# Normalising a tile's hidden values ahead of, and not behind, splitting the next attention pair

## The chip, the cores and the metric

The kernel runs on one core of a Trainium2 chip. Its engines work in parallel, each through its own list of instructions in order: TensorE (PE; PEld is its weight load), VectorE (DVE), ScalarE (ACT), GpSimd (POOL), and SyncE (SP), which issues the DMAs. They meet through semaphores. The metric is the device time of one execution in microseconds, median of several.

## The reference

Windowed attention, then two gated layers, all in fp32:

```python
# attention: 2 batches, 8 heads, 768 positions, head size 64
scores = scale * q @ k.T + bias            # kept: 8 global keys and 96 local ones
a = softmax(scores); attn_out = a @ v
# layer 1: x is [1536, 512], w_in [512, 1024], w_out [1024, 512]
h = x @ w_in
solu = h * softmax(h)
ln = (solu - mean(solu)) / sqrt(var(solu) + 1e-6) * g_ln
y = ln @ w_out
# layer 2: w_gate, w_val [512, 1536], w_down [1536, 512]
yn = y / sqrt(mean(y * y) + 1e-6) * rms_g
out = (silu(yn @ w_gate) * (yn @ w_val)) @ w_down
```

## The kernel before

The 1536 rows are 12 tiles of 128 rows. A first stage does attention and layer 1, tile by tile; a second does layer 2 in 6 blocks of two tiles. Each product of fp32 values is made of three products of parts: a value is rounded to a shorter form (`hi`, on ACT), the rest is `lo = value - hi` (on DVE, "split"), and PE adds hi\*hi, hi\*lo and lo\*hi.

In the first stage, `one_tile(t)` on each engine walks over four steps p = 0 to 3, one for each pair of heads. It is software-pipelined by hand: the attention belongs to tile a = t + 1, the hidden layer to tile t, and the layer norm and the second product of layer 1 to tile t - 1. The order of the calls in `one_tile` is the order of each engine's queue; nothing reorders it. Tiles 2 to 7 run in a loop, the others are written out. In tiles 1 and 8 to 11 DVE also splits weights (`split_block`).

What touches the change, on its engines:

- DVE `take_logits(n + 1)` (L974) takes the scores of a pair out of PSUM, adds the bias and finds the row maximum.
- DVE `split_qk(n + 2)` (L951 and L952) makes `k_lo`, and the rest of the queries in `qk_hi`, of the pair after the next. It waits for ACT's rounding (`qk_rounded`). PE's `score_pair` (L1202, L1203) of that pair waits for it (`qk_split`), and opens the next step p on PE.
- DVE `take_variance(t - 1)` at p = 0 ends in a first guess of one over the square root (L1040). POOL's `newton` (L577, L580, L583, three rounds, then L587) refines it on one column and gives the factor `col[:, 7:8]`.
- DVE `apply_norm(t - 1)` (L1045), at p = 1, waits for that factor and normalises `gated`, 128 x 1024, in place.
- PE `turn_ln(t - 1, 0)` (L1271), at p = 2 right behind `score_pair`, transposes `gated`; ACT and DVE (`split_ln`, L1050) then form `ln_hi` and `ln_lo` for the product with `w_out`.
- PE at p = 1 and 2 also makes the hidden products (`ffn_in`, L399 to L401); at p = 3 it transposes `recip_wide` (L1243). `ffn_out` and `mix_pair` (L1230) fill the rest.

Of the kernel before, what the change touches and what calls it, by code (L numbers as in the profile page):

```python
# [41 lines left out]
def fused_kernel(nc, qk_pairs, v_windows, n_global, n_local,  # L42
# [47 lines left out]
    with whole:  # L90
# [205 lines left out]
        def known(t):  # L296
            return isinstance(t, int)

        def settle(engine, t):


            if not known(t):
                engine.sem_inc(settled, 1)

        def is_tile(t):
            return not known(t) or 0 <= t < tiles
# [508 lines left out]
        def _(dve):  # L815
# [129 lines left out]
            def split_qk(n, p):  # L945

                if not is_pair(n):
                    return
                dve.wait_ge(qk_rounded, n + 1)
                hi = qk_hi[:, p % 2].bitcast(F32)  # L950
                nc.vector.tensor_tensor(k_lo[:, p % 2], qk_raw[:, p, 0:KEYS], hi[:, 0:KEYS], ALU.subtract)  # L951
                nc.vector.tensor_tensor(qk_hi[d:, p % 2, KEYS:], qk_raw[d:, p, KEYS:], hi[d:, KEYS:],  # L952
                                        ALU.subtract).then_inc(qk_split, 1)

            def take_logits(n, even, p):

                if not is_pair(n):
                    return
                dve.wait_ge(scores_ready, n + 1)
                if even == 0 and p == 0 and (not known(n) or n > 0):  # L960
                    dve.wait_ge(bias_set, n // (2 * pairs))
                if known(n) and n < pairs:
                    dve.wait_ge(bias_first, 2 * (p + 1))
                if known(n) and n == pairs:
                    dve.wait_ge(bias_others, heads)
                for h in range(2):
                    if not known(n) or n >= 2:
                        dve.wait_ge(probs_ready, 2 * (n - 2) + h + 1)
                    settle(dve, n)
                    head = 2 * p + h  # L970
                    b = bias_even[:, head] if even == 0 else bias[:, 1, head]
                    if known(n) and n < pairs:
                        b = bias[:, 0, head]
                    nc.vector.tensor_tensor_reduce(logits[:, 2 * (p % 2) + h], scores[h][:, 0:WIN], b,  # L974
                                                   -S_SCALE, 3.0e38, ALU.add, ALU.min,
                                                   neg_max[:, even, head:head + 1]).then_inc(logits_ready, 1)

            def invert_sums(a, even):
                dve.wait_ge(probs_ready, heads * (a + 1))
                nc.vector.tensor_scalar(denom[:], exp_sum[:, even], 1e-9, None, ALU.add).then_inc(denom_steps, 1)  # L980
                dve.wait_ge(denom_steps, 3 * a + 1)
                nc.vector.reciprocal(recip[:], denom[:]).then_inc(denom_steps, 1)
                dve.wait_ge(denom_steps, 3 * a + 2)
                if not known(a) or a >= 1:
                    dve.wait_ge(recip_turned, a)
                nc.vector.tensor_copy(recip_wide[:], recip[:].unsqueeze(2).to_broadcast([P, heads, d])
                                      ).then_inc(denom_steps, 1)

            def normalise_x(a):
                dve.wait_ge(recip_copied, a + 1)  # L990
                dve.wait_ge(mixed_ready, pairs * (a + 1))
                nc.vector.tensor_tensor(x[:], mixed[:].rearrange("p (c n) -> p c n", c=pairs), x[:],
                                        ALU.mult).then_inc(x_ready, 1)
# [6 lines left out]
            def max_hidden(t, n):  # L1000
                dve.wait_ge(hidden_ready, N1 * t + n + 1)
                nc.vector.tensor_reduce(h_max[:, n:n + 1], hidden[:, n], AX_X, ALU.max).then_inc(max_steps, 1)
                if n == N1 - 1:
                    dve.wait_ge(max_steps, 3 * t + 2)
                    nc.vector.tensor_scalar(h_neg[:], h_max[:, 0:1], h_max[:, 1:2], -1.0, ALU.max, ALU.mult
                                            ).then_inc(max_steps, 1)
# [18 lines left out]
            def take_variance(t):  # L1025
                at = LN_STEPS * t
                dve.wait_ge(ln_steps, at + 4)
                settle(dve, t)
                nc.vector.bn_aggr(moments[:], stats[:]).then_inc(ln_steps, 1)
                dve.wait_ge(ln_steps, at + 5)  # L1030

                nc.vector.tensor_scalar(col[:, 2:3], moments[:, 1:2], col[:, 1:2], col[:, 1:2],
                                        ALU.mult, ALU.mult).then_inc(ln_steps, 1)
                dve.wait_ge(ln_steps, at + 6)
                nc.vector.tensor_scalar(col[:, 3:4], col[:, 2:3], 1e-6, None, ALU.add).then_inc(ln_steps, 1)
                dve.wait_ge(ln_steps, at + 7)
                nc.vector.tensor_scalar(seed_bits[:, 0:1], col[:, 3:4].bitcast(I32), 1, None,
                                        ALU.logical_shift_right).then_inc(ln_steps, 1)
                dve.wait_ge(ln_steps, at + 8)
                nc.vector.tensor_scalar(seed_bits[:, 1:2], seed_bits[:, 0:1], -1.0, RSQRT_SEED,  # L1040
                                        ALU.mult, ALU.add).then_inc(seed_ready, 1)

            def apply_norm(t):
                dve.wait_ge(rstd_ready, t + 1)
                nc.vector.tensor_scalar(gated[:], gated[:], moments[:, 0:1], col[:, 7:8],  # L1045
                                        ALU.subtract, ALU.mult).then_inc(ln_ready, 1)

            def split_ln(t, n):
                dve.wait_ge(ln_rounded, N1 * t + n + 1)
                nc.vector.tensor_tensor(ln_lo[:, n * KJ:(n + 1) * KJ], turned_x[:].rearrange("p (k n) -> p k n", k=KJ),  # L1050
                                        ln_hi[:, n * KJ:(n + 1) * KJ].bitcast(F32),
                                        ALU.subtract).then_inc(ln_split, 1)
# [42 lines left out]
            def one_tile(t, even):  # L1095
                a = t + AHEAD
                for p in range(pairs):
                    n = pairs * a + p
                    if p == 0 and is_tile(t):
                        normalise_x(t)  # L1100
                    if p == 3 and is_tile(t):
                        max_hidden(t, 1)
                    take_logits(n + 1, 1 - even if p < pairs - 1 else even, (p + 1) % pairs)
                    if p == 3 and is_tile(a):
                        invert_sums(a, 1 - even)
                    if p == 0 and is_tile(t - 1):
                        take_variance(t - 1)
                    if p == 2 and is_tile(t - 1):
                        split_ln(t - 1, 0)
                    if p == 2 and is_tile(t):  # L1110
                        max_hidden(t, 0)
                    split_qk(n + 2, (p + 2) % pairs)
                    if p == 1 and is_tile(t - 1):
                        apply_norm(t - 1)
                    if p == 0 and is_tile(t):
                        split_x(t, even)
                    if known(t) and t == tiles - 1 and p == 2:
                        normalise_y(0, 0)
                    if p == 2 and is_tile(t - 1):
                        split_ln(t - 1, 1)  # L1120
                    if known(t) and t == tiles - 1 and p == 3:
                        split_y(0, 0, 0)
                    if p == 3 and is_tile(t):
                        gate_hidden(t)
                        measure_hidden(t)
                    if known(t) and t == -AHEAD and p == 0:
                        start_distance(1)
                        finish_distance(1)
                    if known(t) and t == tiles - 4 and p == 1:
                        scale_of_y(0)  # L1130
                    if known(t) and t == tiles - 1 and p == 3:
                        split_y(0, 1, 0)
                        take_variance(t)
                    for c, half in split_1.get((t, p), ()) if known(t) else ():
                        split_block(dve, c, half)
# [340 lines left out]
```

## Time and profile before

| | us |
|---|---|
| median of three runs (597.48 to 598.37) | 598.06 |
| the profiled execution's own time | 598.06 |
| its span, first to last instruction | 596.2 |
| PE busy | 555.7 |
| DVE busy | 308.3 |
| ACT busy | 264.8 |
| POOL busy | 84.4 |

Busy times are of one profiled execution. The first stage lasts until about 275 us in it, the second from there to the end. In a timeline, a bracket behind a row gives how long the engine was idle before it and whose end released it. A busy time of PE counts overlapping matmuls once.

### The profile page before, as it was taken

The page shows a single profiled execution, that of the slowest core. Times are in us where ns is not written, and L with a number is a line of the kernel's source. Part 1 is how long each engine was busy: PE and PEld are TensorE (multiplying, and loading weights), DVE is VectorE, ACT ScalarE, POOL GpSimd, SP SyncE. Part 2 cuts the span into 40 slices and gives each one's busy share as a digit, 9 for nine tenths or more (in the row PEclk, how much of TensorE's full clock was granted, in tenths as well). Part 3 has the DMA queues.
Part 4 walks back from the last instruction along what each step waited for, and adds up shares of the span by engine and source line. Part 5 has one row for each costly group of instructions (what it writes and reads, how often), then busy time and mean ns, then how long its engine had stood idle before and what let it go on. Part 6 is the DMA issues. An engine that isn't in the chain of part 4 may idle for free.

```text
span 596.2 us, 10724 instructions
## 1 busy us (share of the span) xinstructions
PE 555.7 (93%) x3696; PEld 479.1 (80%) x3696; DVE 308.3 (52%) x798; ACT 264.8 (44%) x609; POOL 84.4 (14%) x215
## 2 busy tenths in 40 slices
PE   2368899999999999999999999999999999999997
PEld 1246677777777777768899999999999999999996
DVE  5578788778877898767455213222222222231211
ACT  2557656766776777656454212221222222222112
POOL 1240220322122205323010010001001000100000
PEclk9969799999999999999999999999999999999999
DMA  7767564433443333232532100010020000001000
GB/s 171 190 169 169 155 176 123 124 108 91 123 124 110 92 123 100 94 119 81 184 108 89 48 25 1 1 70 1 1 70 0 0 0 35 0 0 37 2 1 35
DMA packets 22965, 46.95 MB, mean 79 GB/s; under 512 B 4128, under 2 KB 4128, under 8 KB 22928
## 3 DMA queue, kind: packets, MB, share of 16 engines
q1 hardware_dynamic: 22928, 46.48, 26.8%
q8 instruction: 20, 0.33, 0.2%
q14 instruction: 17, 0.14, 0.1%
HBM read 40.18 MB, written 6.29 MB: 78 GB/s over the span
## 4 chain that ended last, share of the span: by engine, by line
PE 79%; DVE 9%; POOL 3%; issue 3%; DMA 3%; ACT 2%; SPq 1%; DVEq 0%; ACTq 0%
PE hidden L399 9%; PE hidden L400 8%; PE hidden L401 8%; PE mixed L1230 4%; PE turned L399 3%; PE scores_a L399 3%; PE mixed L399 3%; PE turned L400 3%; PE scores_b L399 3%; PE mixed L400 3%; PE turned L401 3%; PE scores_a L400 3%; PE scores_b L400 3%; PE scores_b L401 3%; PE scores_a L401 3%
## 5 line engine op out<-in xcount | busy, mean ns | idle before, releaser
L718 ACT ACTIVATE act_hi<-act_sb 128x256 fp32r<-128x256 f32 x72 | 30.1, 418 | 108.3 <-DVE act_sb L1087 108.3
L1087 DVE TENSOR_TENSOR act_sb<-mixed,silu 128x256 f32<-128x256 f32 x36 | 15.3, 425 | 93.9 <-PE mixed L401 93.5
L1087 DVE TENSOR_TENSOR act_sb<-turned,silu 128x256 f32<-128x256 f32 x36 | 15.3, 424 | 89.1 <-PE turned L401 86.5
L399 PE MATMUL hidden<-down_hi,act_hi 128*128 128x512 f32 x144 | 57.1, 397 | 0.1
L400 PE MATMUL hidden<-down_lo,act_hi 128*128 128x512 f32 x144 | 56.9, 395 | 0.0
L401 PE MATMUL hidden<-down_hi,act_lo 128*128 128x512 f32 x144 | 56.7, 394 | 0.0
L662 ACT ACTIVATE probs_t<-turned 116x512 f32<-116x512 f32 x48 | 28.6, 595 | 49.7 <-PE turned L1215 49.6
L1092 DVE TENSOR_TENSOR act_lo<-act_sb,act_hi 128x256 fp32r<-128x256 f32 x72 | 30.6, 425 | 34.9 <-ACT act_hi L718 34.9
L652 ACT ACTIVATE probs<-logits,neg_max 128x232 f32<-128x232 f32 x96 | 45.6, 480 | 3.2 <-DVE neg_max L974 3.2
L1230 PE MATMUL mixed<-probs_t,v_in 116*64 116x128 f32 x384 | 33.9, 301 | 11.9 <-ACT probs_t L662 10.4
L1230 PEld LDWEIGHTS mixed<-probs_t,v_in 116*64 116x64 f32 x384 | 21.6, 145 | 28.7 <-issue 15.1
L642 ACT ACTIVATE qk_hi<-qk_raw 128x720 fp32r<-128x720 f32 x48 | 38.1, 794 | 14.2 <-DMA qk_raw<-qk_pairs 14.2
L399 PE MATMUL hidden<-in_hi,xt_hi 128*128 128x512 f32 x96 | 42.7, 445 | 0.0
L399 PE MATMUL turned<-yt_hi,val_hi 128*128 128x256 f32 x144 | 40.9, 284 | 0.0
L399 PE MATMUL mixed<-yt_hi,val_hi 128*128 128x256 f32 x144 | 40.9, 284 | 0.0
L399 PE MATMUL scores_a<-yt_hi,gate_hi 128*128 128x256 f32 x144 | 40.5, 281 | 0.0
L400 PE MATMUL mixed<-yt_lo,val_hi 128*128 128x256 f32 x144 | 40.4, 281 | 0.0
L400 PE MATMUL turned<-yt_lo,val_hi 128*128 128x256 f32 x144 | 40.4, 281 | 0.0
L400 PE MATMUL scores_b<-yt_lo,gate_hi 128*128 128x256 f32 x144 | 40.4, 281 | 0.0
L400 PE MATMUL scores_a<-yt_lo,gate_hi 128*128 128x256 f32 x144 | 40.4, 281 | 0.0
L401 PE MATMUL turned<-yt_hi,val_lo 128*128 128x256 f32 x144 | 40.4, 281 | 0.0
L399 PE MATMUL scores_b<-yt_hi,gate_hi 128*128 128x256 f32 x144 | 40.4, 281 | 0.0
(142 smaller groups left out, 1556.1 us busy)
## 6 DMA issues: line engine op xcount, KB each, us to landing
qk_raw<-qk_pairs SPq DMA_DIRECT2D x96, 180.0 KB, 3.3
v_in<-v_windows SPq DMA_DIRECT2D x12, 464.0 KB
staging<-w_gate SPq DMA_DIRECT2D x3, 1024.0 KB, 6.9
staging<-w_val SPq DMA_DIRECT2D x3, 1024.0 KB, 6.9
y_spill<-y_out SPq DMA_DIRECT2D x12, 256.0 KB, 7.6
staging<-w_down SPq DMA_DIRECT2D x3, 1024.0 KB, 5.5
y_in<-y_spill SPq DMA_DIRECT2D x6, 512.0 KB, 4.1
out<-o_sb SPq DMA_DIRECT2D x12, 256.0 KB, 2.1
```

The costliest lines, as they stand in the source:

```text
L399: pe.matmul(acc, hi, other_hi, start=first, stop=False)
L400: pe.matmul(acc, hi, other_lo, start=False, stop=False)
L401: return pe.matmul(acc, lo, other_hi, start=False, stop=last)
L642: nc.scalar.activation(qk_hi[:, p % 2], qk_raw[:, p], ACT.Copy).then_inc(qk_rounded, 1)
L652: nc.scalar.activation(probs[:, p % 2, h], logits[:, 2 * (p % 2) + h], ACT.Exp, bias=neg_max[:, even, head:head + 1], scale=-1.0, accum_ou ...
L662: nc.scalar.activation(probs_t[:, p % 2], turned[0:HALF, :], ACT.Copy).then_inc(probs_t_ready, 1)
L718: nc.scalar.activation(act_hi[:, slot], act_sb[:, slot], ACT.Copy).then_inc(act_rounded, 1)
L1087: nc.vector.tensor_tensor(act_sb[:, slot], val_ps[slot][:, 0:WIDE], silu[:, slot], ALU.mult).then_inc(act_ready, 1)
L1092: nc.vector.tensor_tensor(act_lo[:, slot], act_sb[:, slot], act_hi[:, slot].bitcast(F32), ALU.subtract).then_inc(act_split, 1)
L1230: ins = pe.matmul(mixed[h * d:(h + 1) * d, p * P:(p + 1) * P], v_in[:, even, half, head * d:(head + 1) * d], probs_t[:, p % 2, h, half], s ...
```

## The change

In DVE's `one_tile` the call of `apply_norm(t - 1)` at p = 1 moves from behind `split_qk` to ahead of it. Both still come after `take_logits`, each keeps its own waits, and no other engine's list is touched.

```diff
                     if p == 0 and is_tile(t - 1):
                         take_variance(t - 1)
+                    if p == 1 and is_tile(t - 1):
+                        apply_norm(t - 1)
                     if p == 2 and is_tile(t - 1):
                         split_ln(t - 1, 0)
                     if p == 2 and is_tile(t):
                         max_hidden(t, 0)
                     split_qk(n + 2, (p + 2) % pairs)
-                    if p == 1 and is_tile(t - 1):
-                        apply_norm(t - 1)
```

DVE's list in the loop (tiles 2 to 7), at p = 1, the half with the even tiles' bias; the rows with - are where they stood before, those with + where they stand now:

```order
 L974 ISA logits,neg_max<-scores_b,bias_even 128x232 [waits probs_ready]
 L974 ISA neg_max 128x1
+L1045 TENSOR_SCALAR gated<-gated,moments,col 128x1024 [waits rstd_ready]
 L949 REGISTER_ALU
 L951 TENSOR_TENSOR k_lo<-qk_raw,qk_hi 128x464 [waits qk_rounded]
 L952 TENSOR_TENSOR qk_hi<-qk_raw,qk_hi 64x256
-L1045 TENSOR_SCALAR gated<-gated,moments,col 128x1024 [waits rstd_ready]
 L968 ISA [waits scores_ready]
 L974 ISA logits,neg_max<-scores_a,bias_even 128x232 [waits probs_ready]
```

The instruction that waits for POOL (`rstd_ready`) now stands ahead of the two that split the pair.

DVE's list in tile 9, at p = 1, where weights are split behind it:

```order
 L974 ISA logits,neg_max<-scores_b,bias_even 128x232 [waits probs_ready]
 L974 ISA neg_max 128x1
-L951 TENSOR_TENSOR k_lo<-qk_raw,qk_hi 128x464 [waits qk_rounded]
-L952 TENSOR_TENSOR qk_hi<-qk_raw,qk_hi 64x256
 L1045 TENSOR_SCALAR gated<-gated,moments,col 128x1024 [waits rstd_ready]
+L951 TENSOR_TENSOR k_lo<-qk_raw,qk_hi 128x464 [waits qk_rounded]
+L952 TENSOR_TENSOR qk_hi<-qk_raw,qk_hi 64x256
 L380 SCALAR_TENSOR_TENSOR val_lo<-staging,rms_col,val_hi 128x512 [waits w_rounded]
 L380 SCALAR_TENSOR_TENSOR val_lo<-staging,rms_col,val_hi 128x512
```

The same swap; the weights' split keeps its place behind both. PE's list is the same before and after. A `score_pair` in it, in the loop, as it stands in both:

```order
L1198 ISA [waits qk_split]
L1202 MATMUL scores_a<-qk_hi 128x232 [waits logits_ready]
L1203 MATMUL scores_a<-k_lo,qk_hi 128x232
L1198 REGISTER_ALU
L1202 MATMUL scores_b<-qk_hi 128x232 [waits logits_ready]
L1203 MATMUL scores_b<-k_lo,qk_hi 128x232
```

Nothing moved here; this is the place on PE that waits for what DVE's L952 signals.

## Rows read from the trace of the kernel before

**Rows 1.** The page: busy us (share of the span) xinstructions; then the chain.
```profile
PE 555.7 (93%) x3696; PEld 479.1 (80%) x3696; DVE 308.3 (52%) x798; ACT 264.8 (44%) x609; POOL 84.4 (14%) x215
...
PE 79%; DVE 9%; POOL 3%; issue 3%; DMA 3%; ACT 2%; SPq 1%; DVEq 0%; ACTq 0%
```

**Rows 2.** Windows: start:end, length, busy us of each engine, PEclk, DMA share, GB/s.
```profile
100.00:150.00 50.00, 49.60 (x319) 38.04 (x318) 40.27 (x114) 33.31 (x84) 14.42 (x31) 1.00 0.37 108
```

**Rows 3.** Waits around L1045: its own, then those for its output (us, times).
```profile
  POOL col L587: 17.5, 12
who waited for it (us, times):
  PEld turned_x L1271: 3.4, 3
  PE turned_x L1271: 2.4, 3
```

**Rows 4.** Timeline of DVE, tile 5: start us, us, operation, [idle before <-releaser].
```profile
146.42 0.64 DVE L951 TENSOR_TENSOR k_lo<-qk_raw,qk_hi 128x464 fp32r<-128x464 f32 x1
147.07 0.42 DVE L952 TENSOR_TENSOR qk_hi<-qk_raw,qk_hi 64x256 fp32r<-64x256 f32 x1
148.78 0.81 DVE L1045 TENSOR_SCALAR gated<-gated,moments,col 128x1024 f32<-128x1024 f32 x1 [1.28 <-POOL col L587]
```

**Rows 5.** Timeline of POOL, tile 5, and the same steps beside idle DVE, tile 11.
```profile
146.54 0.67 POOL L583 TENSOR_SCALAR col<-col 128x1 f32<-128x1 f32 x1
147.31 0.40 POOL L577 TENSOR_SCALAR col<-col 128x1 f32<-128x1 f32 x1
147.80 0.19 POOL L580 TENSOR_SCALAR col<-col 128x1 f32<-128x1 f32 x1
...
263.15 0.28 POOL L583 TENSOR_SCALAR col<-col 128x1 f32<-128x1 f32 x1
263.54 0.33 POOL L577 TENSOR_SCALAR col<-col 128x1 f32<-128x1 f32 x1
263.96 0.19 POOL L580 TENSOR_SCALAR col<-col 128x1 f32<-128x1 f32 x1
```

**Rows 6.** Timelines of DVE and PE: start-up, then PE in tile 5.
```profile
62.80 0.42 DVE L952 TENSOR_TENSOR qk_hi<-qk_raw,qk_hi 64x256 fp32r<-64x256 f32 x1
...
63.28 0.56 PE L1202 MATMUL scores_a<-qk_hi 128*128 128x232 f32 x1 [1.40 <-DVE qk_hi L952]
...
149.45 0.38 PE L1202 MATMUL scores_a<-qk_hi 128*128 128x232 f32 x1
...
150.00 0.60 PE L1271 MATMUL turned_x<-ident,gated 128*128 128x128 f32 x4
```

**Rows 7.** Timelines of DVE and PE, tile 1, at the swapped place.
```profile
67.65 0.81 DVE L1045 TENSOR_SCALAR gated<-gated,moments,col 128x1024 f32<-128x1024 f32 x1 [1.12 <-POOL col L587]
...
69.64 0.38 PE L1202 MATMUL scores_a<-qk_hi 128*128 128x232 f32 x1
```

**Rows 8.** Timelines of DVE and PE, tiles 8 to 10.
```profile
207.93 0.81 DVE L1045 TENSOR_SCALAR gated<-gated,moments,col 128x1024 f32<-128x1024 f32 x1 [0.84 <-POOL col L587]
...
211.85 0.66 PE L1271 MATMUL turned_x<-ident,gated 128*128 128x128 f32 x4 [0.41 <-DVE ln_lo L1050]
...
228.90 0.81 DVE L1045 TENSOR_SCALAR gated<-gated,moments,col 128x1024 f32<-128x1024 f32 x1 [1.66 <-POOL col L587]
229.63 1.41 DVE L380 SCALAR_TENSOR_TENSOR val_lo<-staging,rms_col,val_hi 128x512 fp32r<-128x512 f32 x2
230.95 0.39 DVE L974 CUSTOM_DVE_ANT_0 logits<-scores_a,bias_even 128x232 f32<-128x232 f32 x1
...
229.77 0.66 PE L1271 MATMUL turned_x<-ident,gated 128*128 128x128 f32 x4 [0.70 <-DVE gated L1045]
...
248.56 0.81 DVE L1045 TENSOR_SCALAR gated<-gated,moments,col 128x1024 f32<-128x1024 f32 x1 [1.11 <-POOL col L587]
```

## The prediction

> **What bounds the kernel now.** I first read the page's busy times and its chain of waits [rows 1]: TensorE (PE) is busy 93% of the span and holds 79% of the chain that ended last, VectorE (DVE) 9%, GpSimd (POOL) 3%. Then the windows, to see whether that holds where the change is made: between 100 and 150 us PE is busy 49.60 of 50 us, at a granted clock of 1.00, DVE 40.27 of 50 [rows 2]. So in the steady tiles PE has almost no holes, and any hole that the change opens in PE's stream is added to the time, while a microsecond saved on DVE alone is worth nothing. The third view is who waits around the moved instruction [rows 3]: before the 12 runs of `apply_norm` DVE stands idle for 17.5 us in all, each time until POOL's last Newton operation, L587. PE and its weight load wait for what `apply_norm` writes only at three places each, 2.4 and 3.4 us. The reader should see that `apply_norm` starts when POOL lets it, not when DVE gets to it.
>
> The timeline of tile 5 shows how that looks [rows 4]. DVE starts the key split (`k_lo`) at 146.42, its second half `qk_hi` at 147.07, and is through at 147.07 + 0.42 = 147.49. Then it idles 1.28 us, and `apply_norm` runs from 148.78 for 0.81. PE takes the product of the pair just split at 149.45 and the transposes of `gated` at 150.00 [rows 6]. So the split is done 149.45 - 147.49 = 1.96 us before PE wants it: this is the slack that the change spends.
>
> **The change, part by part.** Nothing is added or removed. The two split instructions go behind the wait for POOL and behind `apply_norm`, in tiles 1 to 10, ten times (in tile 11 no pair is left to split). Queued behind the wait on DVE are then the split, through it PE's next `score_pair`, and behind that on PE the transposes, the products with `w_in` and everything else, since PE works in order. Where the code prepares weights (tiles 1 and 8 to 10), the splits of those are behind it on DVE too.
>
> *When does `apply_norm` start now?* Were POOL not to change, at the same 148.78, since it was waiting already. But POOL's chain has two stretched places while the split runs beside it [rows 5]: from the L583 at 146.54 to the next start at 147.31 is 0.77 us, and on to 147.80 is 0.49. The same two steps where DVE is idle (263.15 to 263.54 to 263.96) take 0.39 and 0.42. After the change DVE is idle during them, so I take 0.38 + 0.07 = 0.45 us off. The bounds are zero (DVE's split was not what stretched them) and 1.07 (the whole length of the split, 147.49 - 146.42). I take 0.45, since it is a difference of rows of the very same two steps. So `apply_norm` starts at 148.78 - 0.45 = 148.33.
>
> I use starts of consecutive POOL instructions, not their durations. The Trainium skill (Perfetto Trace Analysis, GPSIMD Engine Instruction) advises exactly that, calling the profiled span of a GpSimd instruction unreliable; here the durations in the same rows would give 0.39 + 0.07 = 0.46, so nothing hangs on it.
>
> *When does PE get the pair?* The instruction after `apply_norm` starts 0.73 us after it (228.90 to 229.63 [rows 8]). The split takes 1.07 as above. From its end to PE's start is 0.06: in the start-up stretch, where PE did wait for it, `qk_hi` ended at 62.80 + 0.42 = 63.22 and PE began at 63.28 [rows 6]. So PE starts 0.73 + 1.07 + 0.06 = 1.86 us after `apply_norm` starts: 148.33 + 1.86 = 150.19, against 149.45. That is +0.74 us.
>
> *Does it come back later in the tile?* PE's loss at this place moves PE's later products, DVE's logits that wait for them, the hidden products and with these the sums, the seed and POOL's next Newton chain by the same amount; I see no clock in the loop that runs on by itself (its DMA loads are a tile ahead). The waits of PE for `recip_wide` move with PE's own scores. So nothing is given back in tiles 2 to 7, six tiles alike: 6 x 0.74 = 4.4 us.
>
> *Tile 1.* PE takes its pair at 69.64 while `apply_norm` started at 67.65 [rows 7]. Even with no relief on POOL, 67.65 + 1.86 = 69.51 is before 69.64: cost zero. The cover is 0.13 us, and with POOL's relief some 0.6.
>
> *Tiles 8 to 10.* Here DVE also rounds off weights for the next stage, and is nearly as late as PE. `apply_norm` is at 207.93, 228.90 and 248.56; in tile 9 two weight splits follow at 229.63 and the logits at 230.95 without a pause [rows 8]. What stands behind the swapped group moves by the split's 1.07 less POOL's 0.45, that is 0.62 us. PE meets its pair some 0.9 to 1.1 us later, but it had holes there already, 0.41 us at 211.85 (on `ln_lo`) and 0.70 at 229.77 (on `gated`), which swallow the difference. What passes through is DVE's 0.62: 3 x 0.62 = 1.9 us. The bounds are zero (holes and DVE slack take it all) and 1.07 each.
>
> *Sum.* 0 + 4.4 + 1.9 = 6.3 us on a profiled span of 596.2. The profiled execution took 598.06, which is also the median of the runs shown, with 1.86 outside the span. So 598.06 + 6.3 = 604.4 us, or +1.1%.
>
> **The rivals.**
>
> *POOL is not relieved.* If the stretched steps have another cause, `apply_norm` stays at its times, and tiles 2 to 7 cost 148.78 + 1.86 - 149.45 = 1.19 each, tiles 8 to 10 1.07 each: 7.1 + 3.2 = 10.3, so 608.4 us. For it: POOL's other long steps don't all sit beside a split. Against it: the same steps in the stretch with idle DVE are short. Chance 0.10.
>
> *The late tiles absorb theirs.* Then only 4.4 us remain: 602.5. For it: DVE and PE both have holes in tiles 8 to 10. Chance 0.08.
>
> *POOL is relieved by the whole split.* Tiles 2 to 7 would cost 1.19 - 1.07 = 0.12 each, the late ones nothing: 0.7 us, so 598.8 and no measurable change. Against it: the two steps are stretched by 0.45 in all, and a relief can't give back more than was taken. Chance 0.03. The Trainium skill (SBUF — State Buffer, Who interferes with whom) has a DVE instruction with two SBUF inputs, as both splits are, contend with a GpSimd instruction that reads SBUF, the loser of a shared port blocking fully rather than sharing; were POOL held for all of the split, this rival would follow, but the rows show it held for less than half.
>
> *Faster.* If POOL's result were there by the time DVE has its logits, 146.42, `apply_norm` would not wait, PE's transposes would find `gated` earlier, and DVE would lose its holes of the late tiles (0.84, 1.66 and 1.11 us before the three rows of `apply_norm` [rows 8]). That is 3.6 us at most, since PE hides DVE's holes elsewhere: 594.5. It decides at a relief of 148.78 - 146.42 = 2.36 us on POOL, and against the 0.45 seen there is no sign of it; already for a tie in the steady tiles 1.19 would be needed. Chance 0.02. That the order isn't changed at all is out: DVE's program shows the swap at all its places, with PE's untouched.
>
> *More than that.* Something behind PE's hole could add to it (a weight load not hidden, ScalarE's queue of exponentials getting late). The nearest row is the transposes after a wait, 0.66 us at 229.77 against 0.60 at 150.00: below 0.1 us a tile, which carries it to 605.3. The chance for a time beyond 608.4 I put at 0.04.
>
> **How the numbers follow.** The forecast, 604.4, has 0.73; its own range is 603.4 to 605.8. The range that holds the time 8 times in 10 takes in the late tiles absorbed at its lower end (602.5, a little below for rounding: 602.2) and reaches toward the unrelieved POOL at its upper end (608.4): 602.2 to 608.4. A measurement of this kernel can tell about 0.2%, 1.2 us, from no change. Only the fully relieved POOL lies within it, 0.03; only its early result is faster, 0.02; the rest, 0.95, is slower.
>
> **What would show it.** Right: in tiles 2 to 7 the wait of `k_lo` disappears behind `apply_norm`, DVE's idle before `apply_norm` grows from 1.28 to about 148.33 - 146.42 = 1.9 us, PE shows a hole of 0.7 us before `score_pair` of the last pair, released by `qk_hi` L952, in about nine tiles, and POOL's steps L583 and L577 take 0.39 and 0.42. Wrong: no such hole (the split is still in time), POOL's steps as long as before (then 608), or a later wait in the tile, such as the one for `recip_wide`, shrinking by what PE lost.

## The result, and the profile after

| | before | changed |
|---|---|---|
| median, us | 597.77 (597.32 to 598.37) | 604.23 (604.19 to 604.97) |
| profiled execution, span, us | 596.2 | 603.7 |
| PE busy, us | 555.7 | 557.3 |
| DVE busy, us | 308.3 | 308.5 |
| POOL busy, us | 84.4 | 79.1 |

The changed kernel takes 1.011 of the time before, 95% interval 1.0093 to 1.0128. The forecast was 604.4, and slower. The profiled execution of the changed kernel took 605.45, 1.2 us over its median; the section after the experiments says what such differences are.

The page of the changed kernel, busy times and chain, to be held against [rows 1]:

```profile
PE 557.3 (92%) x3696; PEld 480.5 (80%) x3696; DVE 308.5 (51%) x798; ACT 264.8 (44%) x609; POOL 79.1 (13%) x215
...
PE 65%; DVE 15%; POOL 8%; issue 6%; DMA 3%; ACT 1%; SPq 1%; DVEq 0%; ACTq 0%; POOLq 0%
```

No engine has more than 1.6 us of work added (PE), but the chain no longer stays on PE: its share falls from 79% to 65%, and DVE and POOL rise from 9% and 3% to 15% and 8%. That is what it looks like when two side engines become links of the loop. Where PE had hardly any holes [rows 2] it has them now; the same window (length, busy us of PE, PEld, DVE, ACT, POOL, clock, DMA share, GB/s):

```profile
100.00:150.00 50.00, 48.00 (x303) 36.94 (x304) 40.21 (x114) 32.13 (x80) 11.76 (x27) 1.00 0.37 104
```

PE is busy 48.00 us in place of 49.60 at the same clock. The holes are in one place of each tile. Tile 5 of the changed kernel in the timelines of DVE, POOL and PE, answering to [rows 4 to 6]:

```profile
151.73 0.81 DVE L1045 TENSOR_SCALAR gated<-gated,moments,col 128x1024 f32<-128x1024 f32 x1 [1.81 <-POOL col L587]
152.46 0.64 DVE L951 TENSOR_TENSOR k_lo<-qk_raw,qk_hi 128x464 fp32r<-128x464 f32 x1
153.11 0.42 DVE L952 TENSOR_TENSOR qk_hi<-qk_raw,qk_hi 64x256 fp32r<-64x256 f32 x1
...
149.94 0.28 POOL L583 TENSOR_SCALAR col<-col 128x1 f32<-128x1 f32 x1
150.33 0.33 POOL L577 TENSOR_SCALAR col<-col 128x1 f32<-128x1 f32 x1
150.75 0.19 POOL L580 TENSOR_SCALAR col<-col 128x1 f32<-128x1 f32 x1
...
152.26 0.66 PE L1230 MATMUL mixed<-probs_t,v_in 116*64 116x128 f32 x8
153.66 0.37 PE L1202 MATMUL scores_a<-qk_hi 128*128 128x232 f32 x1 [0.74 <-DVE qk_hi L952]
```

Read from the bottom: PE idles 0.74 us until `qk_hi`; that split ends at 153.11 + 0.42 = 153.53, and it stood behind `apply_norm`, which had waited 1.81 us for POOL. The split itself needed nothing of POOL. POOL's two steps take 0.39 and 0.42 us from start to start, against 0.77 and 0.49 in [rows 5].

What PE loses here is a little more than the bracket says. In the kernel before, the scores of this pair (149.45 in [rows 6]) stood behind

```profile
148.86 0.66 PE L1230 MATMUL mixed<-probs_t,v_in 116*64 116x128 f32 x8
```

that is 0.59 us from start to start. Now it is 153.66 - 152.26 = 1.40, 0.81 more. The bracket of 0.74 counts from the end of the `mixed` products in the record, 0.66 after their start.

Two stretches of PE's timeline measure the cost without the start-up: A from the scores of step 1 of tile 2 to those of step 1 of tile 8, which holds the six swaps of the loop, and B from there to the first transposes of the last tile's `gated`, which holds the three late ones and all that follows in the first stage. The three ends in the kernel before, then in the changed one:

```profile
85.14 0.37 PE L1202 MATMUL scores_a<-qk_hi 128*128 128x232 f32 x1
203.87 0.38 PE L1202 MATMUL scores_a<-qk_hi 128*128 128x232 f32 x1
284.20 0.66 PE L1271 MATMUL turned_x<-ident,gated 128*128 128x128 f32 x4 [0.67 <-DVE gated L1045]
```
```profile
86.09 0.37 PE L1202 MATMUL scores_a<-qk_hi 128*128 128x232 f32 x1
209.74 0.38 PE L1202 MATMUL scores_a<-qk_hi 128*128 128x232 f32 x1
291.62 0.66 PE L1271 MATMUL turned_x<-ident,gated 128*128 128x128 f32 x4 [0.66 <-DVE gated L1045]
```

A went from 118.73 to 123.65, that is +4.92 or 0.82 a tile, and B from 80.33 to 81.88, +1.55. Together 6.5 us, as the medians have it (604.23 - 597.77 = 6.46); the second measurement of the same kernel (e12 below) has 6.2 in A and B and 7.4 by the medians. What follows B, to the end, is 312.0 us before and 312.1 after: nothing comes back. The same two stretches, read in the same way, in all kernels:

| kernel | A, us | B, us | median - median before, us |
|---|---|---|---|
| before | 118.73 | 80.33 | |
| changed, first | 123.65 | 81.88 | +6.5 |
| e12_changed_again | 123.66 | 81.65 | +7.4 |
| e1_loop | 123.62 | 80.33 | +6.4 |
| e2_late | 118.76 | 83.47 | +4.8 |
| e3_first | 118.75 | 80.40 | +0.8 |
| e10_tiles_8_10 | 118.73 | 81.42 | +0.5 |
| e11_tile_9 | 118.72 | 80.90 | +1.1 |
| e4_two_inputs | 125.53 | 83.49 | +10.2 |
| e5_one_input | 123.55 | 81.89 | +7.1 |
| e6_after_two_rounds | 118.71 | 76.96 | -2.4 |
| e7_before_two_rounds | 118.74 | 76.29 | -2.7 |
| e8_turn_first | 121.63 | 81.70 | +3.8 |
| e9_weights_first | 118.79 | 82.01 | +4.0 |

### The profile page after: what moved, and what is told of

It reads as the page before. It is cut to its first block, busy times and chain, and to the rows that moved or that the text cites. A ratio compares the mean times of both kernels' runs of the same rounds, so it can differ in the third digit from the quotient of the medians.

```text
span 603.7 us, 10724 instructions
## 1 busy us (share of the span) xinstructions
PE 557.3 (92%) x3696; PEld 480.5 (80%) x3696; DVE 308.5 (51%) x798; ACT 264.8 (44%) x609; POOL 79.1 (13%) x215
## 4 chain that ended last, share of the span: by engine, by line
PE 65%; DVE 15%; POOL 8%; issue 6%; DMA 3%; ACT 1%; SPq 1%; DVEq 0%; ACTq 0%; POOLq 0%
PE hidden L399 8%; PE hidden L400 7%; PE hidden L401 7%; POOL col L577 3%; PE turned L399 3%; PE mixed L399 3%; PE turned L401 3%; PE turned L400 3%; PE mixed L400 3%; PE scores_b L399 3%; PE scores_a L399 3%; PE scores_b L400 3%; PE scores_a L400 3%; PE scores_a L401 3%; PE scores_b L401 3%
## 5 line engine op out<-in xcount | busy, mean ns | idle before, releaser
L1230 PE MATMUL mixed<-probs_t,v_in 116*64 116x128 f32 x384 | 34.0, 301 | 11.7 <-ACT probs_t L662 10.2
L401 PE MATMUL scores_b<-yt_hi,gate_lo 128*128 128x256 f32 x144 | 40.4, 280 | 0.0
```

The lines of the kernel that those rows point to most:

```text
L401: return pe.matmul(acc, lo, other_hi, start=False, stop=last)
L1230: ins = pe.matmul(mixed[h * d:(h + 1) * d, p * P:(p + 1) * P], v_in[:, even, half, head * d:(head + 1) * d], probs_t[:, p % 2, h, half], s ...
```

## The experiments

### Which tiles pay: the swap in parts

The swap was made under a condition, here for the loop; the others have `known(t) and t >= 8`, `t == 1`, `t in (8, 10)` and `t == 9`:

```diff
+                    if p == 1 and is_tile(t - 1) and (not known(t)):
+                        apply_norm(t - 1)
 ...
                     split_qk(n + 2, (p + 2) % pairs)
+                    if p == 1 and is_tile(t - 1) and not (not known(t)):
+                        apply_norm(t - 1)
```

> The swap in tiles 2 to 7 alone (the loop). My theory: each tile costs PE what it lost in the changed kernel's trace, a hole of 0.74 us before the last pair's scores and a distance of 0.82 us from tile to tile, so 6 x 0.82 = 4.9 us over the kernel before, about +0.8%, and nothing comes back later. Rival, recovery: tiles 8 to 11 have holes of their own (0.41, 0.70 and 0.98 us on PE) and swallow up to 2.1 us of it: +2.8 to 3 us.

Measured: 604.02 against 597.64 us, ratio 1.01 (1.0084 to 1.0116). In the trace A is 4.89 us longer and B is that of before. Six tiles cost 0.82 each and none of it is recovered. The median says 6.4, 1.5 more; in the traced execution these 1.5 lie ahead of the swapped tiles, in the start-up (below).

> The swap in tile 1 alone. My theory: no cost, the split is still done before TensorE wants it; 0.0 us, at most 0.2 either way. Rival: the 0.29 us by which tile 1 was longer in the changed kernel's trace belong to the swap: +0.3 us. (In that trace another 0.67 us had gone by before tile 1, in the start-up, where nothing was changed; I hold that for the difference of two executions.)

Measured: 598.41 against 597.64, ratio 1.0009 (0.9999 to 1.0019), with A and B within 0.1 us of before. Its `apply_norm` started at 67.29 and the split ended at 69.09, and PE took its scores at 69.96 without a wait. Tile 1 costs nothing: the cover held.

> The swap in tiles 8 to 10 alone. My theory: VectorE's split of 1.07 us comes behind the wait, less what POOL is relieved, 0.5 to 0.6 us a tile in the changed kernel's trace, so +1.6 us, about +0.27%. Rival, absorbed: the holes that TensorE had there take it, and the time is that of before within 0.3 us. Rival, TensorE's holes count in full (0.73, 1.71 and 0.75 us before the scores in the changed kernel's trace): +3.2 us.

Measured: 602.44 against 597.64, ratio 1.0075 (1.0062 to 1.0089). Here the theory missed: B is 3.14 us longer, and not 1.55 as in the changed kernel, whose code for these tiles is the same. The whole difference is in tile 9. The rows of this run, PE in tile 9:

```profile
231.01 0.37 PE L1204 MATMUL scores_a<-qk_hi 128*128 128x232 f32 x1 [1.71 <-DVE qk_hi L952]
...
231.60 1.06 PE L1273 MATMUL turned_x<-ident,gated 128*128 128x128 f32 x4
232.31 0.78 PE L399 MATMUL hidden<-in_hi,xt_hi 128*128 128x512 f32 x1
232.88 0.63 PE L400 MATMUL hidden<-in_lo,xt_hi 128*128 128x512 f32 x1
```

and its windows, where the granted clock is the third number from the end:

```profile
231.00:232.00 1.00, 0.98 (x6) 0.99 (x7) 1.00 (x2) 0.00 (x0) 0.84 (x3) 0.75 0.00 0
232.00:233.00 1.00, 1.00 (x6) 0.90 (x5) 1.00 (x5) 0.31 (x1) 0.82 (x3) 0.50 0.70 181
233.00:234.00 1.00, 1.00 (x4) 0.81 (x3) 0.72 (x4) 0.98 (x2) 0.67 (x5) 0.50 1.00 288
```

PE's hole of 0.70 us on `gated` in tile 9 [rows 8] is gone, one of 1.71 us stands before the scores, and behind it the granted clock is 0.50 (1.2 in place of 2.4 GHz): the same products take 0.63 us in place of 0.39. In the changed kernel's first profile the hole was 1.71 us as well, and the clock stayed at 1.00:

```profile
237.50:238.50 1.00, 1.00 (x7) 0.83 (x6) 1.00 (x4) 0.75 (x2) 0.82 (x3) 1.00 0.61 190
```

Three more runs take this apart.

> The swap in tiles 8 and 10 alone, to take apart the run with the swap in tiles 8 to 10, which cost 4.8 us by the medians where 1.6 was expected, and in whose trace TensorE ran tile 9's hidden products after a hole of 1.71 us at a granted clock of 0.50. Theory now: the extra is that stretch at half clock, and it belongs to tile 9's hole. So here there is no such stretch: 0.57 + 0.44 = 1.0 us over the kernel before, a granted clock of 1.00 all through 200 to 300 us. Rival: each of the three late swaps costs some 1.5 us: +3.0 us.

> The swap in tile 9 alone. Theory: a hole of about 1.7 us on TensorE before the last pair's scores, which costs 0.54 us as such, and, where the granted clock falls to 0.50 behind it, 1.6 us more: +2.1 us in those executions. Rival, no clock in it: +0.5 us. Rival, a third of the 4.8 us: +1.6 us without a stretch at 0.50.

> The changed kernel again, with the swap at all ten places. In its first profiled execution tile 9's hole was 1.71 us too, but the granted clock stayed at 1.00 behind it. Theory: six tiles at 0.82 and three late ones at 0.52 us, 6.5 us over the kernel before (604.1 to 604.6), and whether the clock falls in tile 9 differs from execution to execution; where it does, 1.6 us more. Rival: the parts add up (6.4 us for the loop and 4.8 us for the late tiles by the medians), 11 us, and the first measurement was a lucky one.

Measured: 598.85, 599.53 and 605.82 against 598.39 us; ratios 1.0009 (1.0 to 1.0017), 1.001 (1.0001 to 1.002) and 1.0113 (1.0096 to 1.013). In the traces B is 1.09 us longer with tiles 8 and 10, 0.57 with tile 9 alone, and 1.32 with all, none with a stretch at 0.50. The rival by which the parts add up to 11 us has fallen. Tile 9 alone, with the hole and without the fall:

```profile
231.18 0.37 PE L1204 MATMUL scores_a<-qk_hi 128*128 128x232 f32 x1 [1.68 <-DVE qk_hi L952]
...
232.40 0.39 PE L400 MATMUL hidden<-in_lo,xt_hi 128*128 128x512 f32 x1
```

So a late swap costs about 0.5 us, and the 1.6 us on top are TensorE's clock, which fell behind that hole in two traces (e2_late, e4_two_inputs; holes of 1.71 and 1.69 us) and not in four others (1.71, 1.70, 1.68 and 1.42). What decides it is open, and no two traces of one kernel show both. The mean granted clock of each execution, which is on record without a trace too, hints that one kernel can do both: two executions of e4_two_inputs stand at 0.992 and took 608.89 (the traced one) and 609.34 us, two at 0.994 and took 607.24 and 607.00. The slow stretch of its trace, 239.4 to 242.9 us, lowers such a mean by 0.003.

### What stretches POOL

```diff
+                    if p == 1 and not known(t):
+                        dve.wait_ge(qk_rounded, n + 3)
+                        hi = qk_hi[:, (p + 2) % 2].bitcast(F32)
+                        raw = qk_raw[:, (p + 2) % pairs]
+                        nc.vector.tensor_tensor(spare[:, 0:KEYS], raw[:, 0:KEYS], hi[:, 0:KEYS], ALU.subtract)
+                        nc.vector.tensor_tensor(spare[d:, KEYS:QK], raw[d:, KEYS:], hi[d:, KEYS:], ALU.subtract)
                     if p == 1 and is_tile(t - 1):
                         apply_norm(t - 1)
```

> The changed kernel, plus in tiles 2 to 7 a copy of the pair's split into unused memory (two VectorE subtractions, 128x464 and 64x256, each with two inputs in SBUF) at the place where the split stood before, ahead of the wait for POOL. VectorE was idle there for 1.8 us and the copy takes 1.07, so VectorE has the time. My theory: POOL's steps L583 and L577 are stretched again by 0.45 us as in the kernel before, the normalisation is that much later, and each of six tiles costs 0.45 more: 2.7 us over the changed kernel, some 606.9 us, +1.5% over the kernel before. Rival: POOL's stretched steps had another cause, and the time stays at that of the changed kernel, +1.1%.

and, in its place, one instruction with one input:

```diff
+                        nc.vector.tensor_reduce(spare[:, 0:1], qk_raw[:, (p + 2) % pairs], AX_X, ALU.max)
```

> The changed kernel, plus in tiles 2 to 7 a maximum over 128x720 (one input in SBUF, about 0.95 us) at the place of the extra subtractions of the run with two inputs. My theory: it is the second SBUF input of the split that stretches POOL, so this one leaves POOL's steps at 0.39 and 0.42 us from start to start, and the time stays at the changed kernel's, +1.1%. Rival: any VectorE work beside POOL stretches it, +1.5% as with two inputs.

Measured: 608.07 and 604.98 against 597.89 us, ratios 1.0163 (1.0136 to 1.0189) and 1.0109 (1.0086 to 1.0132). DVE and POOL in tile 5, first with two inputs, then with one:

```profile
150.62 0.64 DVE L1112 TENSOR_TENSOR spare<-qk_raw,qk_hi 128x464 f32<-128x464 f32 x1
151.27 0.42 DVE L1113 TENSOR_TENSOR spare<-qk_raw,qk_hi 64x256 f32<-64x256 f32 x1
...
150.76 0.65 POOL L583 TENSOR_SCALAR col<-col 128x1 f32<-128x1 f32 x1
151.51 0.40 POOL L577 TENSOR_SCALAR col<-col 128x1 f32<-128x1 f32 x1
152.00 0.19 POOL L580 TENSOR_SCALAR col<-col 128x1 f32<-128x1 f32 x1
```
```profile
149.43 0.90 DVE L1110 TENSOR_REDUCE spare<-qk_raw 128x1 f32<-128x720 f32 x1
...
149.57 0.28 POOL L583 TENSOR_SCALAR col<-col 128x1 f32<-128x1 f32 x1
149.96 0.33 POOL L577 TENSOR_SCALAR col<-col 128x1 f32<-128x1 f32 x1
150.38 0.19 POOL L580 TENSOR_SCALAR col<-col 128x1 f32<-128x1 f32 x1
```

Beside two inputs POOL's steps are 0.75 and 0.49 us from start to start, beside one 0.39 and 0.42, as if DVE were idle. That settles the term of 0.45. The two instructions also differ in what they write, 464 values in a partition against one. Writing by itself didn't stretch POOL at another place: in the kernel before, `take_logits` (L974, 145.78 to 146.50), with one input in PSUM, one in SBUF and 232 values written to SBUF, ran beside POOL's L577 and L580, and they took 0.42 and 0.29 us from start to start, as in tile 11 beside an idle DVE. The cost was less than expected: A grew by 125.53 - 123.65 = 1.9 us, not 2.7. PE's hole grew from 0.74 to 1.17 on average, the full 0.43, but in the even tiles a later wait, that of PE's L1243 for `recip_wide`, shrank: from 0.58, 0.31 and 0.30 us in tiles 2, 4 and 6 to 0.21, 0.20 and 0.20. The rest of this run's excess is its half-clock stretch in tile 9 (B is 1.6 longer than the changed kernel's).

### Is it the wait for POOL?

```diff
-                for s in range(NEWTON):
+                for s in range(LN_NEWTON):
```

with LN_NEWTON = 2 in place of NEWTON = 3, so that the normalisation's root has one round less of refinement; first in the changed order, then in the order of before.

> The changed kernel with two Newton rounds on POOL in place of three for the layer norm (one round left out, so the factor is less precise), which brings POOL's result 1.09 us earlier. My theory: the hole of 0.74 us on TensorE is the wait for POOL handed on through the split, so it is gone in all tiles where it was, and the time is that of the kernel before with two rounds within 0.5 us, near 597, not above 598.5. Rival: the cost comes from VectorE's order alone (the split simply later by the 0.81 us of the normalisation): then at least two thirds of the 6.5 us stay, 602 or more.

> The kernel before with two Newton rounds in place of three (one left out). My theory: in tiles 1 to 8 and 10 nobody on the chain waits for POOL, and only TensorE's three holes on the normalised values go (0.70 in tile 9, 0.98 in tile 11, 0.67 after it), so 595.5 to 597.5. Rival: POOL's chain bounds nothing, 597.8 as before. With the run of the changed kernel and two rounds it shows what the swap costs when POOL is early.

Measured: 595.49 and 595.24 against 597.89, ratios 0.9964 (0.9948 to 0.9979) and 0.9952 (0.9934 to 0.997). With POOL's result 1.09 us earlier the swap costs 0.0 us in A (118.71 against 118.74) and 0.7 in B, where tile 9 keeps a hole of 0.60. PE in tile 5 of the changed order with two rounds has no bracket:

```profile
146.25 0.81 DVE L1046 TENSOR_SCALAR gated<-gated,moments,col 128x1024 f32<-128x1024 f32 x1 [0.72 <-POOL col L588]
...
148.46 0.37 PE L1203 MATMUL scores_a<-qk_hi 128*128 128x232 f32 x1
```

DVE still waits 0.72 us there, and nobody minds: the split is done at 148.04 and PE comes at 148.46. The order is harmless where the thing waited for comes early enough. They gain 3.4 and 4.0 us in B over the kernel before, more than the 2.35 that the three holes at `gated` gave reason to expect. In the order of before, the 0.41 on `ln_lo` in tile 8 goes too, and each hole was worth more than its bracket: tile 8 is 0.65 us shorter, tile 9 1.09 for its 0.70, and the rest of B 2.30 for 0.98 + 0.67.

### Giving PE something to do in the hole

```diff
+                    if p == 2 and is_tile(t - 1):
+                        turn_ln(t - 1, 0)
                     score_pair(n + 1, (p + 1) % pairs)
                     if p == 0 and is_tile(t - 2):
                         ffn_out(t - 2, range(4, 6))
-                    if p == 2 and is_tile(t - 1):
-                        turn_ln(t - 1, 0)
```

> The changed kernel, with TensorE's order changed to fit it: at the third step of a tile the four transposes of the normalised values (0.44 us) go ahead of the scores of the last pair. They need the normalisation, which the change puts ahead of the split. My theory: they run in the hole, which shrinks from 0.74 to about 0.3 us, so six tiles gain 0.44 each and tiles 8 to 10 up to as much: 2.6 to 3.9 us less than the changed kernel, 600.3 to 601.6, still above the kernel before. Rival: the scores don't get later but what follows does (VectorE's logits, the rounding on ScalarE of the transposed values), and the gain is under 1 us.

Measured: 602.11 against 598.31, ratio 1.0061 (1.0043 to 1.008). A is 2.0 us shorter than in the changed kernel, B 0.2: the right mechanism, but 2.2 us and not 2.6 to 3.9. PE in tile 5:

```profile
150.72 0.66 PE L1230 MATMUL mixed<-probs_t,v_in 116*64 116x128 f32 x8
151.31 0.66 PE L1271 MATMUL turned_x<-ident,gated 128*128 128x128 f32 x4
152.12 0.37 PE L1202 MATMUL scores_a<-qk_hi 128*128 128x232 f32 x1 [0.16 <-DVE qk_hi L952]
```

The hole is 0.16 in place of 0.74, but the scores come no earlier: 152.12 - 150.72 = 1.40 us behind the start of `mixed`, as in the changed kernel. What is saved is the time that the transposes took behind them. In the changed kernel that was 0.35 us from their start to the next product (154.21 to 154.56), not 0.44; A is 0.34 a tile shorter. The late tiles gain almost nothing, since DVE's order decides there.

### Other work ahead of the wait

```diff
+                    for c, half in split_1.get((t, p), ()) if known(t) and p == 1 else ():
+                        split_block(dve, c, half)
                     if p == 1 and is_tile(t - 1):
                         apply_norm(t - 1)
 ...
-                    for c, half in split_1.get((t, p), ()) if known(t) else ():
+                    for c, half in split_1.get((t, p), ()) if known(t) and p != 1 else ():
```

> The kernel before, with another work put ahead of the wait for POOL: the weight splits that stand behind the normalisation at the second step of tiles 1, 9, 10 and 11, 1.41 us each, run ahead of it instead, where VectorE idled 1.66 and 1.11 us in tiles 9 and 10. The attention pair's split stays in front. My theory: VectorE's idle time is filled with work that nobody waits for, so the change's fault is which work is put behind the wait, not that work is moved around it; TensorE gains up to 0.5 us a tile in tiles 9 and 10, 0.3 to 1.0 us in all, a ratio of 0.998 to 1.000. Rival: these splits read two SBUF tensors too and stretch POOL's chain, the normalisation is later and the gain is gone or turned, +0.5 to +1.5 us.

Measured: 601.62 against 597.64, ratio 1.0068 (1.0053 to 1.0083), the rival's side and beyond it. This was an attempt to beat both kernels, and it failed in the way that the rival named. POOL in tile 9, beside the weights' split (228.10 to 229.52 on DVE):

```profile
227.89 0.40 POOL L577 TENSOR_SCALAR col<-col 128x1 f32<-128x1 f32 x1
228.38 0.53 POOL L580 TENSOR_SCALAR col<-col 128x1 f32<-128x1 f32 x1
229.00 0.67 POOL L583 TENSOR_SCALAR col<-col 128x1 f32<-128x1 f32 x1
```

L580 and L583 take 0.53 and 0.67 where they take 0.19 and 0.28 beside an idle DVE. In tile 11, PE's wait for `gated` is on the path, and with the split of `down_lo` beside POOL `apply_norm` started 5.19 us after the seed's last instruction (262.20 to 267.39) and not 4.22 (260.72 to 264.94). In the trace B is 1.7 us longer; the traced execution was the shortest of six, 600.37 us at a mean granted clock of 0.994. The other five took 600.8 to 603.1 at 0.977 or 0.991, values that no execution of the kernel before has (0.980 to 0.997), so part of the median's 4.0 may be falls of the clock as in e2_late; no trace shows them.

## Why the prediction was right

Point by point, by its own steps:

- **PE has no holes there, so a hole costs its length.** Right in kind: A grew by 0.82 a tile, and the loop's swap alone gave the same A and an unchanged B. That the hole is 0.74 in the profile, as predicted, is chance: the predicted 0.74 was a shift from start to start, which measured 0.81.
- **POOL is relieved by 0.45 us.** Right to the hundredth in tile 5 (0.39 and 0.42 us), and shown by the pair of runs with two inputs and one.
- **PE gets the pair 1.86 us after `apply_norm` starts.** A little short: 153.66 - 151.73 = 1.93. The term that was off is the release, 0.06 by the one row of the start-up stretch; it is 153.66 - 153.53 = 0.13 in the loop. With it the sum for tiles 2 to 7 is 4.9, not 4.4.
- **Nothing comes back.** Right at this size: PE's waits for `recip_wide` in tiles 2, 4 and 6 are 0.58, 0.31 and 0.30 us in the kernel before and in the changed one. With the larger hole (two inputs) they shrank by 0.37, 0.11 and 0.10.
- **Tile 1 is covered.** Right (e3_first).
- **Tiles 8 to 10 cost 0.62 each.** Near: 0.55, 0.54 and 0.46 in the changed kernel. POOL is relieved there by more than the 0.45 taken over from tile 5: from the start of its chain to `apply_norm` it is 4.62, 5.59 and 4.63 us in place of 5.16, 6.21 and 5.38. The prediction's way, the split's 1.07 less the relief, would then give 0.53, 0.45 and 0.32; why PE loses more in tiles 9 and 10 is open. That PE meets its pair 0.9 to 1.1 us later, which the prediction gives without a working, is wrong: the holes there are 0.73, 1.71 and 0.75.

The loop cost 0.5 us more than forecast and the late tiles 0.3 less, and the time before came out 0.3 below the 598.06 that the forecast started from (597.77). So it is luck that 604.4 lies within 0.2 us of 604.23; that the mechanism was right is not. What the prediction didn't foresee is that a hole of 1.7 us can cost more than itself by way of PE's clock. It speaks only of something behind the hole that adds to it, at below 0.1 us a tile; in the changed kernel's two profiles the clock didn't fall there, in two variants it did.

## What the runs showed of the hardware

**The start-up differs from execution to execution.** The changed kernel's two traces stand at 86.09 and 87.52 us at the beginning of A. The five kernels whose tiles up to there are those of before stand at 85.14 (before), 85.42, 86.20, 86.43 and 86.62. Of the 1.48 us between before and e1_loop, 0.9 arise between 43.5 and 50.6 us, where PE is slow after its early waits for longer. PE in tile 0 of the kernel before, and of e1_loop:

```profile
46.67 0.52 PE L401 MATMUL hidden<-in_hi,xt_lo 128*128 128x512 f32 x1
47.38 0.48 PE L399 MATMUL hidden<-in_hi,xt_hi 128*128 128x512 f32 x1
47.69 0.39 PE L400 MATMUL hidden<-in_lo,xt_hi 128*128 128x512 f32 x1
```
```profile
47.93 0.78 PE L399 MATMUL hidden<-in_hi,xt_hi 128*128 128x512 f32 x1
48.51 0.60 PE L400 MATMUL hidden<-in_lo,xt_hi 128*128 128x512 f32 x1
48.93 0.40 PE L401 MATMUL hidden<-in_hi,xt_lo 128*128 128x512 f32 x1
```

The same products are fast again from 47.7 us in one and from 48.9 in the other. The granted clock of 44 to 46 us is 0.50 in the profile of before and 1.00 in that of e1_loop, where a 128x512 product takes 0.63 us all the same: here the length of the products is the better witness. In the traced execution of e1_loop the start-up accounts for all that its time has above A and B. For e2_late it doesn't: its trace began A at 85.42 and took 601.41 us, the shortest of five, and why the others took up to 1.2 more is open. Effects below 2 us are better read from A and B than from a few medians.

**Two SBUF inputs on DVE hold up POOL.** A POOL step of 0.39 us took 0.75 beside a DVE subtraction with both inputs in SBUF, 0.39 beside a reduction with one. The Trainium skill (SBUF — State Buffer, Who interferes with whom) says just this of instructions with two SBUF inputs and of `tensor_reduce`, and these runs agree. The price is less than the length of DVE's work: from the start of POOL's chain to `apply_norm` in tile 5 it was 5.12 us beside the split's 1.07, and 4.66 without it. One SBUF input isn't a safe sign in general: in tile 9 of the kernel before, POOL's step L601 on 128x2 took 0.67 us beside `apply_norm` (L1045, one SBUF tensor, 228.90 to 229.71) and 0.20 us at 231.44.

## What to carry to other kernels

In an in-order queue, an instruction that waits for a slow side chain should stand behind everything that others are waiting for, and not ahead of it, however little work it is: ask of each instruction moved behind a wait who consumes it, and how long before that it was ready. Here 1.96 us of slack met 1.07 us of split, 0.73 of the normalisation and the rest of POOL's chain, and what was short was paid in nine of ten tiles, all but the one where PE came late enough. And an idle stretch of VectorE beside a GpSimd chain isn't free to fill: work with two SBUF inputs put there lengthens the very wait that made the stretch.
